# A state read turned one step later, and a state pass whose chunk splits move between the halves of a step

## The chip, the cores and the metric

The kernel runs on one core of a Trainium2 chip. The metric is the device time of one execution in microseconds (us); lower is better. The kernel before was run three times.

## The reference

Three stages follow each other; all of it is float32.

1. Attention between a sequence `x` (8 batches, 8 heads, 512 tokens, 64 wide) and a state of 32 rows per head: each token reads the states (`xread`), each state row reads the tokens (`sread`). Both are softmax attentions without projections. Together they give 8 x (512 + 32) = 4608 rows of 512.
2. A dense layer pair: `g = max(0.01 * h, h)` with `h = x @ w_in` (512 to 2048), then `g @ w_out` (2048 to 512).
3. A mixture of 8 experts (512 to 1024 to 512, relu) in which each row goes to the one expert of its largest logit; the result is scaled by the softmax weight and by a sigmoid gate.

```
h = x @ w_in ; g = maximum(0.01 * h, h) ; x = g @ w_out
logits = x @ w_gate ; e = argmax(logits) ; eom = sigmoid(x @ w_output_gate)
out = softmax(logits)[e] * eom[e] * (relu(x @ w1[e]) @ w2[e])
```

## The kernel before

**Numbers.** A float32 product is made from three matmuls of rounded parts: each operand is split into a `hi` part (a cast, made by ScalarE) and a `lo` part (operand minus `hi`, made by VectorE). `product` (L506 to L510) issues hi x lo, lo x hi and hi x hi. So each operand costs TensorE nothing, but ScalarE and VectorE one operation each, and TensorE waits for the `lo` part.

**Order of the work.** Each engine has one program written out by hand, and semaphores between them. There are nine layers, `layer(b)`: 0 to 7 are the batches with 512 tokens each, and layer 8 (`b == B`) is the state pass: the 256 state rows that the batches' attention left in `sread`. A layer has 16 steps f = 0 to 15, one for each 128 columns of the 2048. On TensorE a step is `up(b, f)` (or `up_states(f)` in the state pass), then `beside_up(b, f)`, then `down(b, f - 2)`, then `beside_down(b, f)`; after step 15 come down(14) and down(15). The two `beside` functions hold the small work of the neighbouring layers: the attention of the batch a = b + 1 and the routing of the rows of layer r = b - 1. The batches' W_in product is taken with the states first (`make_v`), so that `up` of a layer reads `v_hi`, `v_lo`, `aT_hi`, `aT_lo`; `up_states` has no such short cut and reads W_in itself, in 16 chunks of 128 columns, that are split on the way (`chunk_hi(f)` on ScalarE into `wch_hi`, L959, `chunk_lo(f)` on VectorE into `wch_lo`, L1337). `chunk_hi(f)` may start when up(f - 1) is done, and `up_states(f)` waits for `chunk_lo(f)`.

**The g step.** Behind up(f), ScalarE scales the bank by 0.01 (L937), VectorE takes the max (L1196, `g_ready`), ScalarE casts it into `gT_hi` (L943), and VectorE subtracts into `gT_lo` (L1200, `g_lo_done`), for which down(f) waits. up(f) waits for the max of f - 2. Both engines have a function `g_step`, with a `beside_g` between its halves; `layer` calls it and then does what belongs beside step f. In the state pass that is the routing of layer 7 (`keep_yT`, `keep_parts`, `exp_gates` on ScalarE; `add_logits`, `route`, `sum_gates`, `route_gate`, `route_ranks`, `route_rows`, `route_slots` on VectorE in steps 5 to 10), then the chunk f + 2, and then, in the steps of `FIRST_PIECE_AT` (0, 3, 11, 13), one piece of the first expert's weights (`split_expert`, L977 and L1333).

**The state read.** In step 13 of layer b TensorE makes the state read of batch a = b + 1 (`read_states`, L559) in `aux[0]`. VectorE copies it to `scT` (`keep_read`, L1163), TensorE turns it with two transposes into the other half of `aux[0]` (`turn_read`, L566), and VectorE copies that into `sread` (`keep_sread`, L1168 and L1169, `sread_kept`). For batch 0 this is done in steps 5 and 6 of layer 0. In step 15 TensorE waits for `sread_kept` and makes the next v in the same banks.

**The first expert's rows.** The routing sends the rows into a table in DRAM, ordered by expert. The expert with the most rows so far is chosen in layer 7 (`choose_first`), and GpSimd loads the first 256 of its rows into `xq` (`load_rows`, L413, `rows_in`) when the rows of layers 0 to 6 are in the table. In step 14 of the state pass VectorE waits for them and turns them with two transposes (`turn_quarters`, L1352) into `t_b`, the banks 2 and 3; the state pass uses banks 0 and 1 for its downs. It also copies their scales into `s_next`, which lies in a part of `y_buf` that the scatter of layer 7's rows still reads; that is what the wait for `rows_set` is for. After step 15 ScalarE and VectorE make `xgT_hi` and `xgT_lo` from `t_b` (L968, L1346), and the expert phase begins.

Of the kernel before, what the change touches and what calls it, by code (L numbers as in the profile page):

```python
# [35 lines left out]
def build(nc, xT_in, x_in, stT_in, st_in, w_in, w_out, w_gates, w1, w2, consts, tri_in, slot_init, out):  # L36
# [7 lines left out]
    with ctx:  # L44
# [460 lines left out]
        def _(pe):  # L505
# [163 lines left out]
            def beside_up(b, f):  # L669
# [10 lines left out]
                elif f == 3 and r is None:  # L680
                    flip_a2(0, 0, aux[0])
                elif f == 4 and r is None:
                    flip_a2(0, 1, aux[1])
                elif f == 6 and r is None:
                    turn_read(0)
                elif f == 4 and r is not None:
                    if b < B:
                        pe.wait_ge(v_lo_done, v_count(b, 1, 1))
                    else:
                        pe.wait_ge(yT_ready, 4 * r + 2)  # L690
                    flip_y(r, 3)
                elif f == 14 and a is not None:
                    turn_read(a)

            def beside_down(b, f):
# [44 lines left out]
                elif f == 13 and a is not None:  # L740
                    read_states(a)
                elif f == 15 and a is not None:
                    pe.wait_ge(sread_kept, a + 1)
                    make_v(a, 0)
# [135 lines left out]
        def _(act):  # L880
# [50 lines left out]
            def g_step(b, f):  # L931
# [5 lines left out]
                act.mul(g_buf[:, n, 0:w], up_b[n][:, 0:w], 0.01).then_inc(scaled, 1)  # L937
                beside_g(b, f)
                act.wait_ge(g_ready, u)

# [38 lines left out]
            def layer(b):  # L979
                a, r = b + 1 if b < B - 1 else None, b - 1 if b > 0 else None  # L980
                for f in range(F1):
# [24 lines left out]
                    if b == B - 1 and f == F1 - 1:  # L1006
                        chunk_hi(0)
                    if b == B and f + 2 < F1:
                        chunk_hi(f + 2)
                    if b == B and f in FIRST_PIECE_AT:  # L1010
# [82 lines left out]
        def _(dve):  # L1093
# [98 lines left out]
            def g_step(b, f):  # L1192
# [4 lines left out]
                if b < B - 1:  # L1197
                    beside_g(b + 1, f)
                dve.wait_ge(g_hi_done, u)
                dve.tensor_tensor(gT_lo[f % 4][:, 0:w], g_buf[:, n, 0:w], gT_hi[f % 4][:, 0:w].bitcast(fp32), ALU.subtract).then_inc(g_lo_done, 1)  # L1200
# [147 lines left out]

            def turn_quarters(i):
                dve.wait_ge(rows_in, 80 * i + 80)  # L1350
                for n in range(2):
                    dve.transpose(t_b[n][:, :].rearrange("p (k g t) -> p g k t", k=2, t=NS),  # L1352
                                  xq[:, :, 2 * NS * n:2 * NS * n + 2 * NS].rearrange("p g (k d) -> p g k d", k=2)).then_inc(t_ready, 1)
                if not (isinstance(i, int) and i == 0):
                    dve.wait_ge(s_moved, i)
                dve.wait_ge(t_ready, 2 * i + 2)
                dve.tensor_copy(s_next[:, :].rearrange("p (u o) -> p u o", o=1), s_in[:, :, 0:1]).then_inc(s_taken, 2 if isinstance(i, int) and i == 0 else 1)

            def layer(b):
                a, r = b + 1 if b < B - 1 else None, b - 1 if b > 0 else None  # L1360
                for f in range(F1):
# [43 lines left out]
                    if a is not None:  # L1405
# [3 lines left out]
                        elif f == 13:  # L1409
                            a_lo(a, 1)  # L1410
                            keep_read(a)
                        elif f == 14:
                            keep_sread(a)
                        elif f == 15:
                            v_rest(a, 0)
                    if r is not None and f == (14 if b < B else 10):
                        route_slots(r, 4)
                    if b == B and f == 14:
                        dve.wait_ge(y_kept_a, 2 * B)
                        dve.wait_ge(rows_set, 64 * B)  # L1420
                        turn_quarters(0)
                    if b == B - 1 and f == 0:
# [3 lines left out]
                    if b == B - 1 and f == F1 - 1:  # L1426
                        chunk_lo(0)
                    if b == B and f + 2 < F1:
                        chunk_lo(f + 2)
                    if b == B and f in FIRST_PIECE_AT:  # L1430
# [227 lines left out]
```

## Time and profile before

| | |
|---|---|
| median of 3 runs | 1134.91 us (1133.59 to 1134.99) |
| the profiled execution | 1132.32 us, span 1130.6 us |
| TensorE (PE) busy | 1107.4 us, 98% of the span |
| VectorE (DVE) busy | 624.0 us, 55% |
| ScalarE (ACT) busy | 401.5 us, 36% |
| GpSimd (POOL) busy | 206.9 us, 18% |
| granted TensorE clock, mean | 0.999 of full speed |
| state pass | about 648 to 700 us of the span |

In the rows below, times are us from the start of the span. PE is TensorE's matmuls, DVE VectorE, ACT ScalarE, POOL GpSimd. L508 is line 508 of the kernel. A timeline row has start, duration, engine, line, operation, what it writes and reads, sizes and the number of instructions merged; in brackets stands how long the engine was idle before it, and what released it. Matmuls overlap: one of 512 columns is shown as 0.39 us long, but the next starts 0.23 us after it, so distances are taken from start to start.

### The profile page before, as it was taken

How to read it: one execution, taken by the hardware profiler on the slowest of the kernel's cores; microseconds unless marked ns; L12 is line 12 of the kernel's file. 1: busy time of each engine (PE TensorE's matmuls, PEld its weight loads, DVE VectorE, ACT ScalarE, POOL GpSimd, SP SyncE). 2: the span in 40 equal slices, each digit the busy share in tenths (PEclk: the TensorE clock that was granted, in tenths of full speed). 3: DMA queues.
4: the chain of work that ended last, by engine and by line, in shares of the span. 5: the costliest groups of instructions: out<-in, count | busy, mean ns of one | idle time of the engine just before them, and what ended most of it. 6: DMA issues, size and time to landing. Idle time of an engine off the chain costs nothing.

```text
span 1130.6 us, 18025 instructions
## 1 busy us (share of the span) xinstructions
PE 1107.4 (98%) x6514; PEld 895.5 (79%) x6515; DVE 624.0 (55%) x1365; ACT 401.5 (36%) x752; POOL 206.9 (18%) x297
## 2 busy tenths in 40 slices
PE   6999999999999999999999999999999999999997
PEld 2777777777777777777777888998998988889895
DVE  6684574664754854844844566745333335467242
ACT  4344334334434433443343355333111124154121
POOL 1100011020020020110110303532222232443231
PEclk9999999999999999999999999999999999999999
DMA  9398297495693891940030301277111112645110
GB/s 339 130 287 242 76 279 213 126 281 159 181 291 95 233 284 52 289 127 1 38 75 1 131 2 38 86 196 189 46 46 56 37 60 70 178 102 146 41 54 23
DMA packets 73010, 149.87 MB, mean 133 GB/s; under 512 B 11232, under 2 KB 12512, under 8 KB 72929
## 3 DMA queue, kind: packets, MB, share of 16 engines
q1 hardware_dynamic: 59696, 115.34, 36.5%
q0 software_dynamic: 13248, 33.71, 10.3%
q8 instruction: 36, 0.59, 0.2%
q14 instruction: 30, 0.24, 0.1%
HBM read 131.11 MB, written 92.01 MB: 197 GB/s over the span
## 4 chain that ended last, share of the span: by engine, by line
PE 90%; DVE 5%; DMA 2%; issue 1%; ACT 1%; POOL 0%; DVEq 0%; SPq 0%; ACTq 0%; POOLq 0%
PE bank L508 28%; PE bank L510 27%; PE bank L509 26%; PE bank L541 3%; PE bank L559 2%; DMA raw<-w_dram 1%; PE bank L575 1%; DVE w_lo L1333 1%; PE bank L583 1%; PE bank L519 1%; PE bank L548 1%; DMA XT<-xT_in_dram 0%; DVE g_buf L1196 0%; PE bank L793 0%; DVE gT_lo L1200 0%
## 5 line engine op out<-in xcount | busy, mean ns | idle before, releaser
L508 PE MATMUL bank<-wout_lo,gT_hi 128*128 128x512 f32 x544 | 215.9, 397 | 1.4 <-DVE gT_lo L1200 0.9
L510 PE MATMUL bank<-wout_hi,gT_hi 128*128 128x512 f32 x544 | 212.3, 390 | 0.0
L509 PE MATMUL bank<-wout_hi,gT_lo 128*128 128x512 f32 x544 | 212.0, 390 | 0.0
L1196 DVE TENSOR_TENSOR g_buf<-g_buf,bank 128x512 f32<-128x512 f32 (+1 forms) x144 | 94.2, 655 | 102.9 <-ACT g_buf L937 100.8
L508 PE MATMUL bank<-xgT_lo,w_hi 128*128 128x256 f32 x512 | 144.7, 283 | 0.6 <-DVE w_lo L1333 0.5
L510 PE MATMUL bank<-xgT_hi,w_hi 128*128 128x256 f32 x512 | 143.8, 281 | 0.0
L509 PE MATMUL bank<-xgT_hi,w_lo 128*128 128x256 f32 x512 | 143.8, 281 | 0.0
L937 ACT ACTIVATE g_buf<-bank 128x512 f32<-128x512 f32 (+1 forms) x144 | 82.5, 573 | 150.0 <-PE bank L510 148.3
L1200 DVE TENSOR_TENSOR gT_lo<-g_buf,gT_hi 128x512 fp32r<-128x512 f32 (+1 forms) x144 | 95.4, 662 | 72.9 <-ACT gT_hi L943 70.9
L404 POOL DMA_INDIRECT rows_dram<-y_buf,row_i x34 | 35.0, 1030 | 543.2 <-DVE row_i L1290 535.5
L943 ACT CAST gT_hi<-g_buf 128x512 fp32r<-128x512 f32 (+1 forms) x144 | 85.9, 597 | 134.3 <-DVE g_buf L1196 132.6
L1034 ACT ACTIVATE hT_hi<-bank 128x256 fp32r<-128x256 f32 x128 | 49.1, 383 | 220.6 <-PE bank L510 218.3
L508 PEld LDWEIGHTS bank<-wout_lo,gT_hi 128*128 128x128 f32 x544 | 102.2, 188 | 28.1 <-DVE gT_lo L1200 6.4
L510 PEld LDWEIGHTS bank<-wout_hi,gT_hi 128*128 128x128 f32 x544 | 102.1, 188 | 22.4
L509 PEld LDWEIGHTS bank<-wout_hi,gT_lo 128*128 128x128 f32 x544 | 102.3, 188 | 20.2
L508 PE MATMUL bank<-w_lo,hT_hi 128*128 128x512 f32 x296 | 116.4, 393 | 0.7
L510 PE MATMUL bank<-w_hi,hT_hi 128*128 128x512 f32 x296 | 115.5, 390 | 0.0
L509 PE MATMUL bank<-w_hi,hT_lo 128*128 128x512 f32 x296 | 115.5, 390 | 0.0
L508 PE MATMUL bank<-aT_lo,v_hi 128*128 128x512 f32 x254 | 107.9, 425 | 0.8 <-DVE v_lo L1178 0.2
L1463 DVE SCALAR_TENSOR_TENSOR hT_lo<-bank,hT_hi 128x256 fp32r<-128x256 f32 x128 | 53.4, 424 | 87.4 <-ACT hT_hi L1034 83.7
L510 PE MATMUL bank<-aT_hi,v_hi 128*128 128x512 f32 x254 | 100.1, 394 | 0.0
L509 PE MATMUL bank<-aT_hi,v_lo 128*128 128x512 f32 x254 | 99.7, 392 | 0.0
(217 smaller groups left out, 1740.8 us busy)
## 6 DMA issues: line engine op xcount, KB each, us to landing
rows_dram<-x_in_dram SPq DMA_DIRECT2D x17, 4128.0 KB
xq<-rows_dram POOLq DMA_DIRECT2D x88, 128.0 KB, 2.9
raw<-w_dram SPq DMA_DIRECT2D x20, 512.0 KB
raw<-w_dram SPq DMA_DIRECT2D x10, 1024.0 KB
X<-x_in_dram SPq DMA_DIRECT2D x8, 1024.0 KB
XT<-xT_in_dram SPq DMA_DIRECT2D x7, 1024.0 KB, 5.7
win<-w_in_dram SPq DMA_DIRECT2D x4, 1024.0 KB, 13.0
y_buf<-w_out_dram POOLq DMA_DIRECT2D x6, 512.0 KB, 6.5
```

Source lines behind the costliest of these rows:

```text
L404: pool.indirect_dma_start(out=rows_dram, out_offset=bass.IndirectOffsetOnAxis(ap=row_i[:, t:t + 1], axis=0), in_=y_buf[:, t, :], in_offset ...
L508: pe.matmul(o, l_hi, r_lo, start=first, stop=False)
L509: pe.matmul(o, l_lo, r_hi, start=False, stop=False)
L510: return pe.matmul(o, l_hi, r_hi, start=False, stop=last)
L541: last = pe.matmul(to[g][NS * c:NS * c + NS, :], stT[b % 2][rows, c, cols], win[rows, c, VW * k:VW * k + VW], start=True, stop=True)
L559: last = pe.matmul(aux[0][D * i:D * i + D, P * u:P * u + P], a_flat[:, q:q + 2 * NS], X[:, t, P * c:P * c + P], start=(t == 0), stop=(t == 3))
L937: act.mul(g_buf[:, n, 0:w], up_b[n][:, 0:w], 0.01).then_inc(scaled, 1)
L943: act.copy(gT_hi[f % 4][:, 0:w], g_buf[:, n, 0:w]).then_inc(g_hi_done, 1)
L1034: act.activation(hT_hi[:, f, :], h_b[f % 4][:, :PAIR], ACT.Relu).then_inc(h_hi_done, 1)
L1196: dve.tensor_tensor(g_buf[:, n, 0:w], g_buf[:, n, 0:w], up_b[n][:, 0:w], ALU.max).then_inc(g_ready, 1)
L1200: dve.tensor_tensor(gT_lo[f % 4][:, 0:w], g_buf[:, n, 0:w], gT_hi[f % 4][:, 0:w].bitcast(fp32), ALU.subtract).then_inc(g_lo_done, 1)
L1463: dve.scalar_tensor_tensor(hT_lo[:, f, :], h_b[f % 4][:, :PAIR], 0.0, hT_hi[:, f, :].bitcast(fp32), ALU.max, ALU.subtract).then_inc(h_lo_d ...
```

## The change

Three edits.

1. `turn_read(a)` for the batches 1 to 7 moves from `beside_up(b, 14)`, ahead of down(12), to `beside_down(b, 14)`, behind it. On VectorE `route_slots` now comes ahead of `keep_sread` in step 14.
2. In the state pass (the first `g_step` of the diff is ScalarE's, the second VectorE's) `chunk_hi(f + 2)` moves from the end of step f into ScalarE's `g_step`, between the scaling and the cast, and `chunk_lo(f + 2)` into VectorE's, between the max and gT_lo.
3. `turn_quarters` is divided into `turn_tiles` and `take_scales`. In the state pass the transposes of the first expert's rows are done at the end of step 4, the scales are still taken in step 14. Elsewhere `turn_quarters` calls both.

```diff
             def beside_up(b, f):
...
-                elif f == 14 and a is not None:
-                    turn_read(a)
...
             def beside_down(b, f):
...
                     read_states(a)
+                elif f == 14 and a is not None:
+                    turn_read(a)
...
             def g_step(b, f):
...
                 beside_g(b, f)
+                if b == B and f + 2 < F1:
+                    chunk_hi(f + 2)
                 act.wait_ge(g_ready, u)
...
-                    if b == B and f + 2 < F1:
-                        chunk_hi(f + 2)
...
             def g_step(b, f):
...
                     beside_g(b + 1, f)
+                if b == B and f + 2 < F1:
+                    chunk_lo(f + 2)
                 dve.wait_ge(g_hi_done, u)
...
-            def turn_quarters(i):
+            def turn_tiles(i):
                 dve.wait_ge(rows_in, 80 * i + 80)
                 for n in range(2):
                     dve.transpose(...).then_inc(t_ready, 1)
+
+            def take_scales(i):
                 if not (isinstance(i, int) and i == 0):
                     dve.wait_ge(s_moved, i)
                 dve.wait_ge(t_ready, 2 * i + 2)
                 dve.tensor_copy(s_next[...], s_in[:, :, 0:1]).then_inc(s_taken, ...)
+
+            def turn_quarters(i):
+                turn_tiles(i)
+                take_scales(i)
...
-                        elif f == 14:
+                    if r is not None and f == (14 if b < B else 10):
+                        route_slots(r, 4)
+                    if a is not None:
+                        if f == 14:
                             keep_sread(a)
                         elif f == 15:
                             v_rest(a, 0)
-                    if r is not None and f == (14 if b < B else 10):
-                        route_slots(r, 4)
                     if b == B and f == 14:
-                        dve.wait_ge(y_kept_a, 2 * B)
                         dve.wait_ge(rows_set, 64 * B)
-                        turn_quarters(0)
+                        take_scales(0)
...
-                    if b == B and f + 2 < F1:
-                        chunk_lo(f + 2)
+                    if b == B and f == 4:
+                        dve.wait_ge(y_kept_a, 2 * B)
+                        turn_tiles(0)
```

## Rows read from the trace of the kernel before

**Rows 1.** TensorE's waits of the whole span: engine, line, releaser: us, times, longest.
```profile
PE bank L566 <- DVE scT L1163: 0.9, 5, 0.2
PE bank L508 <- DVE gT_lo L1200: 0.9, 1, 0.9
PE bank L508 <- DVE wch_lo L1337: 0.7, 2, 0.5
```
**Rows 2.** Timeline of TensorE around the turned state read, layer 6.
```profile
560.62 0.39 PE L510 MATMUL bank<-aT_hi,v_hi 128*128 128x512 f32 x1
561.16 0.44 PE L566 MATMUL bank<-const,scT 128*128 128x128 f32 x2 [0.15 <-issue]
...
561.67 0.39 PE L509 MATMUL bank<-wout_hi,gT_lo 128*128 128x512 f32 x1
```
**Rows 3.** Timeline of TensorE around the same transposes, layer 0.
```profile
85.16 0.39 PE L510 MATMUL bank<-aT_hi,v_hi 128*128 128x512 f32 x1
85.39 0.38 PE L566 MATMUL bank<-const,scT 128*128 128x128 f32 x2
...
85.84 0.40 PE L509 MATMUL bank<-wout_hi,gT_lo 128*128 128x512 f32 x1
```
**Rows 4.** Timeline of VectorE, layer 6, the copy before the transposes.
```profile
560.68 0.42 DVE L1163 COPY scT<-bank 128x256 f32<-128x256 f32 x1 [2.16 <-PE bank L559]
```
**Rows 5.** Timeline of TensorE in the state pass, around its stalls.
```profile
652.12 0.35 PE L508 MATMUL bank<-sr_lo,wch_hi 128*128 128x256 f32 x1 [0.50 <-DVE wch_lo L1337]
...
655.22 0.40 PE L510 MATMUL bank<-wout_hi,gT_hi 128*128 128x512 f32 x1
655.62 0.35 PE L508 MATMUL bank<-sr_lo,wch_hi 128*128 128x256 f32 x1
...
672.07 0.39 PE L510 MATMUL bank<-wout_hi,gT_hi 128*128 128x512 f32 x1
672.52 0.36 PE L508 MATMUL bank<-sr_lo,wch_hi 128*128 128x256 f32 x1
...
678.15 0.39 PE L510 MATMUL bank<-wout_hi,gT_hi 128*128 128x512 f32 x1
678.74 0.35 PE L508 MATMUL bank<-sr_lo,wch_hi 128*128 128x256 f32 x1 [0.20 <-DVE wch_lo L1337]
678.93 0.28 PE L509 MATMUL bank<-sr_hi,wch_lo 128*128 128x256 f32 x1
...
696.99 0.39 PE L510 MATMUL bank<-wout_hi,gT_hi 128*128 128x512 f32 x1
698.31 0.50 PE L508 MATMUL bank<-wout_lo,gT_hi 128*128 128x512 f32 x1 [0.93 <-DVE gT_lo L1200]
```
**Rows 6.** Timeline of ScalarE, step 0 of the state pass.
```profile
649.45 0.38 ACT L937 ACTIVATE g_buf<-bank 128x256 f32<-128x256 f32 x1 [0.81 <-PE bank L510]
650.32 0.41 ACT L943 CAST gT_hi<-g_buf 128x256 fp32r<-128x256 f32 x1 [0.49 <-DVE g_buf L1196]
650.63 0.62 ACT L959 CAST wch_hi<-win 128x512 fp32r<-128x512 f32 x1
```
**Rows 7.** Timeline of VectorE in the state pass: chunks, a split, the row transposes.
```profile
651.28 0.69 DVE L1337 TENSOR_TENSOR wch_lo<-win,wch_hi 128x512 fp32r<-128x512 f32 x1
...
683.53 0.69 DVE L1337 TENSOR_TENSOR wch_lo<-win,wch_hi 128x512 fp32r<-128x512 f32 x1
...
693.08 1.23 DVE L1333 TENSOR_TENSOR w_lo<-raw,w_hi 128x1024 fp32r<-128x1024 f32 x1 [0.26 <-issue]
...
695.45 1.31 DVE L1352 STREAM_TRANSPOSE bank<-xq 128x512 f32<-128x512 f32 x2
```
**Rows 8.** GpSimd: row loads, a row scatter, and the loads' landing (queries xq, timeline).
```profile
645.05 2.40 POOL L413 DMA_DIRECT2D xq<-rows_dram  x4
...
682.83 1.02 POOL L404 DMA_INDIRECT rows_dram<-y_buf,row_i  x1 [0.31 <-issue]
...
DMA to landing us min/median/max: 2.7/2.8/2.9
```

## The prediction

> **What bounds the kernel now.** I read the list of TensorE's waits first, because in a kernel whose matmul engine is busy all the time only what stops that engine can be won. In the eight layers it names one repeated wait, that of the two state-read transposes for the copy that feeds them, 0.9 us in five places; in the state pass it names one for gT_lo (0.9 us) and two for wch_lo (0.7 us) [rows 1]. The other waits of that list lie in the first 75 us or in the expert phase, where the diff changes nothing. So TensorE sets the end, and the question is how much of its time between these places is stall. A wait costs more than its idle number, because the matmuls behind it start anew; I therefore read the timeline of TensorE at each place and take distances from start to start. An undisturbed 512-column matmul is followed by the next instruction 0.23 us after its start (85.16 to 85.39) [rows 3].
>
> **Part one, the state read.** Now TensorE runs up(14), then the transposes, then down(12). The copy L1163 that they need starts at 560.68 and takes 0.42 us [rows 4], while the last matmul of up(14) has already started at 560.62; the transposes start at 561.16. From that last up matmul to the second down matmul there are 561.67 - 560.62 = 1.05 us [rows 2]. Layer 0 shows the same four instructions without a wait (there the copy was early): 85.84 - 85.16 = 0.68 us [rows 3]. The difference, 0.37 us, is the price of one wait with its restart. The transposes stand in seven layers (0 to 6); layer 0 already pays nothing, so six remain: 6 x 0.37 = 2.2 us. Their idle time is 0.15 us in layer 6, but 0.9 us over the five others, 0.18 each [rows 1, 2], so I add 5 x 0.03 and round to **2.4 us**.
>
> After the change the transposes come behind down(12), 12 matmuls of 0.23 us (2.7 us) later than now, when the copy has long ended: nothing waits, and the two transposes cost what layer 0 shows. What is moved by this: the copy into sread on VectorE waits for them. VectorE first does route_slots, which has been put ahead of it and has nothing to do with the transposes; its eight small operations now stand behind the copy. The copy must be over before TensorE's make_v of step 15, another up and down (12 + 6 matmuls, over 4 us) behind the transposes, and before VectorE's own max of step 15. I cost it at nothing; its cover is that up and down. If it were gone, the two copies (under 1 us) would stall TensorE once a layer.
>
> **Part two, the state pass.** One step is 12 matmuls of 256 columns and 6 of 512, about 2.8 us. Five stalls are in the diff's reach [rows 5]:
> up(2) idles 0.50 us for its chunk;
> 655.62 - 655.22 = 0.40, less 0.23, is 0.17;
> 672.52 - 672.07 = 0.45, so 0.22;
> 678.74 - 678.15 = 0.59, so 0.36;
> 698.31 - 696.99 = 1.32, so 1.09, before the last down.
> Together 2.34 us. After a wait the next start is late too: 678.93 - 678.74 = 0.19 where half of 0.23 would do, 0.07 us more. Five times that is 0.35. Sum 2.7 us; since the first stall follows transposes, its own restart may be dearer, and I take **2.8 us**, with 2.3 (idle alone) and 3.0 as bounds.
>
> Are they removed? The first four are chunks that come late. ScalarE starts the scaling of step 0 at 649.45, casts g at 650.32 and only then the chunk at 650.63; VectorE subtracts it from 651.28 and TensorE starts at 652.12 [rows 5, 6, 7]. Between the chunk's two halves there are 0.65 us, from the second to TensorE 0.84, and from one ScalarE operation of this size to the next 0.31. In the new order the chunk starts right behind the scaling: 649.45 + 0.31 + 0.65 + 0.84 = 651.25, and TensorE comes there at 652.12 - 0.50 = 651.62, or, if the restart is counted in, some 0.2 earlier. So it is just in time; this is the tightest place, and a remainder of 0.1 or 0.2 us is possible. The other chunks have more: since the chunk now goes ahead of what a step does beside it (the route, the gates, the splits of the first expert, 1.23 us each [rows 7]), it is ready some 1.8 us after the scaling starts, while TensorE needs it only after two downs and an up, over 4 us. Those side jobs no longer hold up a chunk, only the next max.
>
> The last stall has another cause. Around 693 to 698 VectorE is one queue: a split of 1.23 us from 693.08, max and gT_lo of step 14, then the two transposes of the first expert's rows, 1.31 us from 695.45, and only then max and gT_lo of step 15, for which TensorE waits 1.09 us [rows 5, 7]. The change takes the 1.31 us out of this queue and moves it to step 4; only the small copy of the scales stays. 1.31 is more than 1.09, and the split before it also comes earlier, because the chunk ahead of it does; so the whole stall goes.
>
> What it adds: a step's cast and gT_lo now stand behind the chunk on their engines. On VectorE the chunk's 0.69 us comes between max and gT_lo, of which some 0.5 us was spent waiting for the cast; gT_lo is 0.2 us later, 0.7 us where ScalarE also copies a transposed y. The down that reads it is two steps away, more than 3 us of room; in steps 14 and 15 there is no chunk at all. I cost it at nothing. The row transposes at step 4 stand behind gT_lo(4) and ahead of max(5): 1.31 us in a step of 2.8 us that also holds one split; max(5) may be late, but what needs it is up(7). They wait for the rows, whose loads are issued from 645.05 in 2.4 us and land 2.8 us later [rows 8], so by about 651; step 4 is reached after 660. The bound from below is nothing, from above the time by which the loads would be later than 660. Banks and buffers that they write lie unused in this pass. The order of GpSimd's queue is the same; its row scatters start 1 to 2 us earlier with the gates.
>
> **The sum.** 2.4 + 2.8 = 5.2 us. After the state pass each chain that TensorE takes part in starts from it (the last routing, the second rows, the loads of the experts, issued as buffers come free), so the shift should reach the end whole. The profiled execution took 1132.32 us (span 1130.6); it would be 1127.1. It is 2.6 us below the median of the runs shown; from the median 1134.91 the same 5.2 us (0.46%) give 1129.7.
>
> **The rivals.**
> *Chunks or turns stay late, one part alone pays.* If the state pass only moves its stalls (each engine does as much as before, and 0.2 us at up(2) is thin), only 2.4 us remain: 1132.5. If instead the transposes behind down(12) make something else in the layer late, 2.8 us remain: 1132.1. For the first speaks that VectorE is fuller here than in a layer; against it that each of the five stalls has its own named operation in front, which is moved.
> *No change that can be told.* The layers and the pass both just move the wait to the next place, for example to gT_lo before a down. The room of over 3 us speaks against it. 1134.9.
> *Slower: the rows aren't there.* At step 4 VectorE waits for the row loads; all that stands behind it (max(5), the chunks) then holds up TensorE. It decides once the loads land later than about 664, 13 us later than the rows say [rows 8]; from there each us costs one, and beyond 5.2 more it is slower than before: with the landing at 675, some 11 - 5 = 6 us, 1141. In the kernel before this would have been hidden, since it waited for them at 695.
> *GpSimd and VectorE block each other.* The row scatters of GpSimd move against VectorE's two-input subtractions. The row says no: a scatter from 682.83 lasts 1.02 us, and the chunk's subtraction at 683.53, inside it, takes 0.69 us as does the one at 651.28 with GpSimd idle [rows 7, 8]. If a new meeting did cost a whole scatter, 1.0 us in a step that also has a split, I would lose about 1 us: 1130.7.
> The Trainium skill, "SBUF — State Buffer", section "Who interferes with whom", has the rule for this rival: a VectorE instruction with two SBUF inputs contends with a GpSimd instruction that reads SBUF, and the loser waits the whole instruction. By that rule the sum would be 4.2 instead of 5.2; the trace does not show it at the one meeting that I read.
>
> **How the numbers follow.** Forecast 0.72; one part alone 0.13; GpSimd's blocking 0.03; no change 0.08; slower 0.04. A change of 0.2% (2.3 us) is about what a measurement of this kernel can tell from none. The forecast and the blocking case are beyond it; one part alone, 2.4 or 2.8 us, comes out beyond it in some seven of ten: faster 0.72 + 0.03 + 0.09 = 0.84, within 0.12, slower 0.04. The range goes from all bounds at their best (2.4 + 3.0, and another 1.3 us, by which the lowest run shown lies under the median) at 1128.2 to one part alone at 1132.6.
>
> **What the profile after would show.** TensorE's waits without the state-read transposes, and 0.68 us in layers 1 to 6 where 1.05 stood, one down later; no wait for gT_lo and at most a short one for wch_lo at up(2); the row transposes on VectorE near 661; the expert phase as before, 5 us earlier. I am wrong if TensorE waits for gT_lo before a down in the state pass, if make_v waits for sread in every layer, or if VectorE idles at step 4 for a load.

## The result, and the profile after

The changed kernel takes 1127.24 us (median of 4 runs, 1126.89 to 1127.44), the kernel before in the same comparison 1134.66 us (4 runs, 1133.59 to 1134.99). The ratio is 0.9938, with a 95% interval of 0.9925 to 0.995: it is 7.4 us faster, 0.6%; in us the interval is 5.7 to 8.5. The forecast was 1129.7 us with a range from 1128.2 to 1132.6, so the time lies below the range. The two profiled executions are 5.4 us apart: 1132.32 to 1126.89 us, spans 1130.6 to 1125.2 us. The one of the changed kernel is one of its four timed runs; that of the kernel before is not among its four and lies 1.3 us below the lowest of them, and whether it ran on the same chip is not known.

First the list of TensorE's waits after the change (releaser, us in total, times, longest), to be laid beside [rows 1]:

```profile
core 0 of [0], span 1125.2 us
PE bank L532 <- DMA stT<-stT_in_dram: 5.3, 1, 5.3
PE bank L616 <- ACT aT_hi L899: 2.4, 2, 2.0
...
PE bank L508 <- DVE w_lo L1335: 0.5, 1, 0.5
PE bank L508 <- DVE hT_lo L1472: 0.3, 1, 0.3
PE bank L541 <- DVE sread L1169: 0.3, 1, 0.3
```

All three rows of [rows 1] are gone: no wait of the transposes for scT, none for wch_lo, none for gT_lo. The wait for sread was there before with the same 0.3 us. One is new, 0.3 us for hT_lo in the expert phase, at 1031.69. It is no mark of the change: later profiles of the kernel before have it too, `control` with 0.4 us and `control_2` with 0.6.

**The state read.** The trace's answer on the sixteen transposes after the change: duration in ns (least, median, most), first and last start, then what ended idle time before them, and who waited for them. Both lists are empty.

```profile
L566 PE MATMUL bank<-const,scT x16: 270/271/273, 44.6 to 561.5; 128*128 128x128 f32 x16
its engine sat idle before it (us, times) until:
who waited for it (us, times):
```

In each of the layers 0 to 6 the last matmul ahead of the transposes and the second down matmul behind them are 0.68 us apart, the distance of [rows 3]. In [rows 2] it was 1.05. But the copy that feeds them is no earlier. VectorE after, layer 6:

```profile
555.63 0.68 DVE L1173 TENSOR_TENSOR aT_lo<-scT,aT_hi 128x512 fp32r<-128x512 f32 x1
559.18 0.42 DVE L1163 COPY scT<-bank 128x256 f32<-128x256 f32 x1 [2.87 <-remote]
559.89 0.69 DVE L1196 TENSOR_TENSOR g_buf<-g_buf,bank 128x512 f32<-128x512 f32 x1 [0.28 <-ACT g_buf L937]
```

The state read begins at 555.25 on TensorE, the copy 3.9 us later, after VectorE had idled for 2.9 us. The late copy now has down(12) in front of its reader.

**The state pass.** (It has 256 rows; with the 8 x 512 of the batches the kernel works on 4352, and the 4608 in the section on the reference is a slip: 8 x (512 + 32) is 4352.) TensorE around up(2), where [rows 5] show a start at 652.12 with 0.50 us of waiting:

```profile
648.34 0.28 PE L510 MATMUL bank<-sr_hi,wch_hi 128*128 128x256 f32 x1
648.46 0.60 PE L575 MATMUL bank<-const,y_buf 128*128 128x128 f32 x4
648.81 0.36 PE L508 MATMUL bank<-sr_lo,wch_hi 128*128 128x256 f32 x1
```

The timeline of ScalarE in that step, which answers to [rows 6]:

```profile
646.89 0.39 ACT L937 ACTIVATE g_buf<-bank 128x256 f32<-128x256 f32 x1 [0.81 <-PE bank L510]
647.17 0.61 ACT L961 CAST wch_hi<-win 128x512 fp32r<-128x512 f32 x1
647.77 0.41 ACT L945 CAST gT_hi<-g_buf 128x256 fp32r<-128x256 f32 x1
```

And that of VectorE, for [rows 7], with step 4 behind it:

```profile
647.31 0.42 DVE L1196 TENSOR_TENSOR g_buf<-g_buf,bank 128x256 f32<-128x256 f32 x1 [0.50 <-ACT g_buf L937]
647.82 0.69 DVE L1339 TENSOR_TENSOR wch_lo<-win,wch_hi 128x512 fp32r<-128x512 f32 x1
...
658.66 0.68 DVE L1339 TENSOR_TENSOR wch_lo<-win,wch_hi 128x512 fp32r<-128x512 f32 x1
659.26 0.42 DVE L1202 TENSOR_TENSOR gT_lo<-g_buf,gT_hi 128x256 fp32r<-128x256 f32 x1
659.60 1.31 DVE L1354 STREAM_TRANSPOSE bank<-xq 128x512 f32<-128x512 f32 x2
661.93 0.42 DVE L1196 TENSOR_TENSOR g_buf<-g_buf,bank 128x256 f32<-128x256 f32 x1 [1.03 <-ACT g_buf L937]
```

The chunk starts 0.28 us behind the scaling (before: 1.18, 649.45 to 650.63) and its second half 0.93 us behind it (before: 1.83). The row transposes run at step 4 without a wait for their rows, and VectorE idles 1.03 us behind them, so they had room. The end of the pass, where [rows 5] show 1.32 us between two starts:

```profile
693.75 0.39 PE L509 MATMUL bank<-wout_hi,gT_lo 128*128 128x512 f32 x1
693.97 0.39 PE L510 MATMUL bank<-wout_hi,gT_hi 128*128 128x512 f32 x1
694.20 0.28 PE L508 MATMUL bank<-xgT_lo,w_hi 128*128 128x256 f32 x1
```

Nothing but steps of 0.23 us, up to the first matmul of the expert phase. So the gain can be read off at fixed places of TensorE's program. The first wait of the kernel's L541 ends 0.26 us earlier (48.32 to 48.06), before any edited place. up(1) of the state pass begins at 646.96 instead of 649.51: 2.55 us, so the seven layers gave 2.29. The expert phase begins at 694.20 instead of 699.82: 5.62, so the state pass gave 3.07. The spans end 5.4 us apart; the expert phase gave 0.2 back, where the profile after has the wait for hT_lo.

By this the working holds against the profiled execution: 2.4 was forecast for the turns and 2.29 came, 2.8 for the pass and 3.07 came, just above its bound of 3.0; 1127.1 was the time and 1126.89 it was. What does not hold is the median: 7.4 us, where the parts give 5.4. The experiments ask where the other 2 us are, and why the copy of the state read is late at all.

### The profile page after: what moved, and what is told of

Its sections match the earlier page's. It is cut to its first block, busy times and chain, and to the rows that moved or that the text cites. A ratio compares the mean times of both kernels' runs of the same rounds, so it can differ in the third digit from the quotient of the medians.

```text
span 1125.2 us, 18025 instructions
## 1 busy us (share of the span) xinstructions
PE 1103.7 (98%) x6514; PEld 895.9 (80%) x6515; DVE 622.4 (55%) x1365; ACT 401.2 (36%) x752; POOL 207.6 (18%) x297
## 4 chain that ended last, share of the span: by engine, by line
PE 91%; DVE 4%; DMA 2%; issue 1%; ACT 1%; POOL 0%; DVEq 0%; SPq 0%; ACTq 0%; POOLq 0%
PE bank L508 29%; PE bank L510 27%; PE bank L509 27%; PE bank L541 3%; PE bank L559 1%; DMA raw<-w_dram 1%; PE bank L575 1%; PE bank L583 1%; PE bank L519 1%; PE bank L548 1%; DVE w_lo L1335 1%; DMA XT<-xT_in_dram 1%; DVE v_lo L1178 0%; PE bank L793 0%; PE bank L590 0%
## 5 line engine op out<-in xcount | busy, mean ns | idle before, releaser
L937 ACT ACTIVATE g_buf<-bank 128x512 f32<-128x512 f32 (+1 forms) x144 | 82.5, 573 | 153.8 <-PE bank L510 152.2
```

## The experiments

Each kernel was timed beside the kernel before on the same chip. The kernels of one table were timed together on one chip, and that is called one comparison here; with the one above there are seven. A median's ratio has an interval of about 0.1% to either side, 1 us.

### The three edits apart (second comparison; before: 1131.46 us, 33 runs)

`control` is the kernel before, unchanged. `turn_only` has edit 1 of the diff, `chunks_only` edit 2, `rows_only` edit 3. Their core:

```diff
 turn_only
-                elif f == 14 and a is not None:      # beside_up
-                    turn_read(a)
+                elif f == 14 and a is not None:      # beside_down
+                    turn_read(a)
 chunks_only
+                if b == B and f + 2 < F1:            # in both g_step
+                    chunk_hi(f + 2)                  # chunk_lo on VectorE
 rows_only
-                        turn_quarters(0)             # step 14
+                        take_scales(0)
+                    if b == B and f == 4:
+                        dve.wait_ge(y_kept_a, 2 * B)
+                        turn_tiles(0)
```

> The kernel before, under another name. Theory A (the gain is 5.4 us, the difference of the two profiled spans, and the other 2 us of the medians is a spread of executions that has nothing to do with the change): the control's own runs spread over 1132 to 1135, ratio 0.9985 to 1.0015, and with five rounds the median of before may come down to 1133. Theory B (the executions of the kernel before without the luck of the profiled one are really 2 us longer, because its stalls are longer there): runs at 1134 to 1135 with few exceptions.

> Only the state read's transposes behind down(12), with route_slots ahead of keep_sread. By the profile 6 x 0.39 = 2.3 us less, TensorE without the wait for L1163; in the medians 2.3 us as well by theory A. By theory B, if the stalls in the layers are what differs between executions, up to 4 us.

> Only the chunk splits between the halves of the g step. The stalls at up(2), up(3), up(8), up(10) go (1.7 us); the wait for gT_lo before the last down stays but is shorter, since the split ahead of the row transposes comes some 0.5 us earlier: 2.0 to 2.4 us less in all. The rival that the stalls move to a down would leave it at 0 to 1 us.

> Only the transposes of the first expert's rows in step 4. The wait before the last down goes, 1.2 us less; the four chunk stalls stay, and the one or two chunks behind step 4 may come later, since they now stand behind 1.31 us of transposes: a gain between 0.7 and 1.2 us. If it interacts with the chunks (max of step 5 late, chunk 7 late) 0 to 0.5 us.

| kernel | median us | ratio, 95% interval | against 1131.46 |
|---|---|---|---|
| control | 1131.68 | 1.0004, 0.9995 to 1.0013 | +0.2 |
| turn_only | 1129.84 | 0.9985, 0.9976 to 0.9994 | -1.6 |
| chunks_only | 1129.36 | 0.9984, 0.9975 to 0.9993 | -2.1 |
| rows_only | 1131.24 | 0.9999, 0.999 to 1.0008 | -0.2 |

`chunks_only` came as expected, the others did not. The kernel before is itself 3.2 us faster here than in the first comparison (1131.46 against 1134.66). `turn_only` gained 1.6 us where 2.3 or more were expected. And the rows' edit, which by [rows 5] should have been worth 1.09 us, is worth nothing that can be told. The end of the state pass of `control` says why:

```profile
696.13 0.39 PE L510 MATMUL bank<-wout_hi,gT_hi 128*128 128x512 f32 x1
696.51 0.50 PE L508 MATMUL bank<-wout_lo,gT_hi 128*128 128x512 f32 x1
```

0.38 us between the starts, so a stall of 0.15 and not of 1.09, in the same program. The stalls of the chunks are as in [rows 5]: 0.75 us at up(2) with its restart, 0.16, 0.21 and 0.36. The turns of the state read are cheaper too: 1.03, 0.94, 0.91, 0.91, 0.95 and 0.95 us in the layers 1 to 6 of `control`, where 0.68 is the undisturbed distance. The excess is 1.6 us, and `turn_only` gains 1.6 in the median (0.7 to 2.7 by its interval); in `turn_only` all seven are 0.68.

### The whole, and the whole less one part (third comparison; before: 1129.74 us, 33 runs)

`full_again` is the changed kernel. `turn_chunks` leaves the rows where they were, `state_only` leaves out edit 1, `turn_no_slots` leaves route_slots behind keep_sread.

```diff
 turn_no_slots, against the changed kernel, VectorE, step 14
-                    if r is not None and f == (14 if b < B else 10):
-                        route_slots(r, 4)
                     if a is not None:
...
+                    if r is not None and f == (14 if b < B else 10):
+                        route_slots(r, 4)
```

> The whole change, timed together with the kernel before. Theory C (the price of the removed waits is that which this chip's executions show, 0.25 us a turn and 0.2 us before the last down where these are as in the control's profile): the parts alone gave 1.6, 2.1 and 0.2 us, so 3.7 to 4.0 us in all. Theory A (5.4 us, as between the first two profiles): 5.2 to 5.6. Theory B (7.4 us, as between the first medians): above 7.

> The change without the early row transposes. Theory C: the two parts add, 3.7 us, and the rows add nothing to it, because the earlier chunks already free the end of VectorE's queue. The rival (the row transposes' 1.31 us at the end of the pass are worth 1 us): 1 us slower than the whole change, with a wait for gT_lo before the last down.

> Chunks and rows without the turned state read. Theory C: as the chunks alone, 2.1 to 2.3 us. The rival that the two help each other (rows at step 4 were held up by late chunks): 3 us or more.

> The whole change, but route_slots stays behind keep_sread on VectorE. By my forecast nothing, within 0.3 us of the whole change, since over 4 us of matmuls lie between the transposes and the make_v that needs the copy. The rival: VectorE waits 0.5 us or so for the later transposes, is late with the max of step 15, and that costs 0.3 us or more in each of six layers, 2 us or more.

| kernel | median us | ratio, 95% interval |
|---|---|---|
| full_again | 1127.68 | 0.9983, 0.9974 to 0.9992 |
| turn_chunks | 1127.89 | 0.9984, 0.9975 to 0.9993 |
| state_only | 1127.59 | 0.9981, 0.9972 to 0.999 |
| turn_no_slots | 1127.75 | 0.9982, 0.9973 to 0.9991 |

The four can't be told apart and are some 2.1 us faster than before; the 3.7 us or more that were expected of `full_again` and `turn_chunks` did not come. On this chip the turned read is worth nothing: `state_only`, which hasn't got it, shows 0.68 us in every layer. The order of route_slots is worth nothing, as costed, and the early row transposes 0.2 us, which can't be told from nothing. And the changed kernel takes 1127.7 us, close to the 1127.2 of the first comparison, while the kernel before has gone from 1134.7 over 1131.5 to 1129.7. What varies from comparison to comparison is the kernel before.

### The cause of the late copy (fourth comparison; before: 1129.46 us, 27 runs)

`control_2` and `full_3` repeat both kernels. `scatter_late` holds back GpSimd's row scatters of the layers 0 to 5 until the state read is kept; `copy_act` lets ScalarE make the copy L1163.

```diff
 scatter_late, GpSimd
-            with pool.Fori(1, B) as blocks:
+            for blocks in range(1, B - 1):
+                pool.wait_ge(sread_kept, blocks + 2)
 copy_act, ScalarE, beside step 13 (VectorE's keep_read(a) is left out)
+                        elif f == 13:
+                            act.wait_ge(sread_ps, a + 1)
+                            act.wait_ge(aT_lo_done, 2 * a + 1)
+                            act.copy(scT[:, 0, 0:2 * P], aux[0][:, 0:2 * P]).then_inc(read_kept, 1)
```

> The kernel before once more, for a profile of it from the chip of this call. In its profiles so far the copy L1163 of layers 1 to 6 starts 3.1 to 3.3 us after the state read's first matmul, while in layer 0, and in every layer of the four kernels of the last call, it starts 2.0 us after. Theory D (the row scatters that GpSimd issues at that moment hold the copy back on some chips and not on others): either 2.0 and no turn stall with a time of before near 1129.7, or 3.1 or more with a stall of 0.25 us or more a turn and a time of 1131 or more. Nothing in between.

> The whole change. Theory D: its own time is 1127.0 to 1127.9 on any chip, since it waits for none of the things that differ; the gain is the kernel before's time less that: 2.0 us where before takes 1129.7, 4 where it takes 1131.5, 7.4 where it takes 1134.7. The rival (chips differ for reasons outside the stalls, and both kernels alike): the gain stays near 2 to 4 whatever the kernel before takes.

> The kernel before, in which GpSimd issues the row scatters of the batches' layers 0 to 5 only after the state read of the layer is kept. Theory D: the copy starts 2.0 us after the first state-read matmul in layers 1 to 6 and the turns cost 0.68 us as in layer 0, on any chip; where the kernel before has the stall, 1.5 to 2.4 us less, otherwise the same time. The rival (the lateness has nothing to do with the scatters): 3.1 us and the stall stay.

> The kernel before, in which ScalarE instead of VectorE copies the read states of layers 0 to 6. If it is VectorE that the scatters hold back, the copy on ScalarE starts 2.0 to 2.1 us after the first matmul in every layer, and the turn stall goes (1.5 to 2.4 us less where it is). If the signal from TensorE is late for everybody, the copy is late on ScalarE too, with the stall unchanged.

| kernel | median us | ratio, 95% interval |
|---|---|---|
| control_2 | 1129.59 | 1.0, 0.999 to 1.0009 |
| full_3 | 1127.36 | 0.9979, 0.997 to 0.9988 |
| scatter_late | 1147.23 | 1.0157, 1.0138 to 1.0175 |
| copy_act | 1130.33 | 1.0007, 0.9998 to 1.0016 |

`full_3` lies in the 1127.0 to 1127.9 us that were expected of it on any chip. This chip, too, has no late copy to cure, and so neither of the two could decide. But it gives the undisturbed picture of the place of [rows 2, 4]. The timeline of TensorE in `control_2`, the kernel before, layer 6:

```profile
555.48 1.75 PE L559 MATMUL bank<-X,a_buf 128*64 128x128 f32 x28
...
558.64 0.39 PE L510 MATMUL bank<-aT_hi,v_hi 128*128 128x512 f32 x1
558.87 0.38 PE L566 MATMUL bank<-const,scT 128*128 128x128 f32 x2
559.01 0.48 PE L508 MATMUL bank<-wout_lo,gT_hi 128*128 128x512 f32 x1
559.32 0.40 PE L509 MATMUL bank<-wout_hi,gT_lo 128*128 128x512 f32 x1
```

And that of VectorE there:

```profile
555.87 0.68 DVE L1173 TENSOR_TENSOR aT_lo<-scT,aT_hi 128x512 fp32r<-128x512 f32 x1
557.50 0.42 DVE L1163 COPY scT<-bank 128x256 f32<-128x256 f32 x1 [0.94 <-PE bank L559]
```

The copy starts 2.02 us behind the first matmul of the read, in this and every other layer; in the first profile it was 560.68 - 557.46 = 3.22 us. In neither is VectorE busy when the read ends: the copy only waits for TensorE's signal. The records of the semaphores say the same from the other side. They hold the time at which each increment was made; from the start of the last matmul of the state read to the increment that releases the copy, the median over the eight reads is

```
kernel before, first profile      1.52 us
kernel before, control            1.38 us
kernel before, control_2          0.30 us
changed kernel, full_again        0.30 us
```

So it is the signal itself that is late, by some 1.2 us, and not VectorE that is busy. (The ends of matmuls are modelled in a profile, so it can't say whether the last matmul's result came late as well; the matmuls behind it started on time.) In the first profile the same holds at v_ps (some 1.2 us late in each of the layers 1 to 6), at the up of one later step of each layer (0.4 us) and at three ups of the state pass, its steps 12 to 14 (1.1, 1.3 and 1.5 us). Of these the timeline of ScalarE shows the last two in the first profile and in `control_2`, at the scaling (L937) that the signal releases. First the kernel before, first profile:

```profile
690.29 0.38 ACT L937 ACTIVATE g_buf<-bank 128x256 f32<-128x256 f32 x1 [1.22 <-PE bank L510]
...
693.31 0.38 ACT L937 ACTIVATE g_buf<-bank 128x256 f32<-128x256 f32 x1 [0.26 <-remote]
```

Then `control_2`, ScalarE as well:

```profile
686.60 0.38 ACT L937 ACTIVATE g_buf<-bank 128x256 f32<-128x256 f32 x1
...
689.56 0.38 ACT L937 ACTIVATE g_buf<-bank 128x256 f32<-128x256 f32 x1
```

The last matmul of up(14) starts at 691.41 in the one and at 689.09 in the other, so the scaling follows 1.90 us behind it in the one and 0.47 in the other. That shifts VectorE's queue at the end of the pass. Its row transposes start at 695.45 [rows 7] in the one, at 692.06 in the other: 3.39 us apart, while TensorE is only 2.4 us apart there. The 1.0 us between is the difference of the last stall: 1.09 us in the first profile, 694.92 - 694.55 - 0.23 = 0.14 in `control_2`. In `control` up(12) and up(14) are late as well, by 1.0 and 0.6 us, but not up(13); its row transposes start where those of `control_2` do, seen from TensorE (693.65, and the matmul ahead of the stall at 696.13), and its last stall is 0.15 us. So of these two profiles the late signals of the pass cost something only in the one in which up(13) is among them.

`copy_act` is 0.9 us above the kernel before, which its interval does not tell from none. `scatter_late` was 17.8 us slower (5 runs) for another reason than the one under test: the next layer's y waits for the late scatters, and TensorE for y.

```profile
184.87 0.63 PE L578 MATMUL bank<-const,y_buf 128*128 128x128 f32 x4 [3.68 <-DVE y_buf L1210]
```

### Are GpSimd's scatters the cause? (three more comparisons)

The late signals fall in the parts of a layer in which GpSimd issues the scatters of rows and slots. GpSimd's timeline in the first profile, layer 6, the last row scatter beside the state read of [rows 4]:

```profile
559.67 0.98 POOL L404 DMA_INDIRECT rows_dram<-y_buf,row_i  x1 [0.30 <-issue]
```

It ends at 560.65; the read's increment, due 0.30 us behind its last matmul at 559.45, is recorded at 560.66, and the copy starts at 560.68. In the other five layers too the increment comes within 0.03 us of the end of a row scatter. Over the whole profile, past its first 30 us, 26 of TensorE's increments are over 0.15 us later than is usual for their semaphore, and each of them is made while GpSimd is at an indirect scatter or within 0.4 us of it (80 of the 615 increments are); the profile after has 21 and `control` 24, all in such places. `no_scatter` leaves those of six layers out, for small ordinary DMAs that raise the same semaphores (the slots' in the same way as the rows' below); part of the table stays empty. `control_3` to `control_5` stand beside it.

```diff
-            with pool.Fori(1, B) as blocks:
-                set_rows(blocks, 4)
-                set_slots(blocks, 4)
+            for b in range(1, B - 1):
+                pool.wait_ge(row_ready, b)
+                for t in range(4):
+                    pool.dma_start(pad_dram[8 * b + t:8 * b + t + 1, :], row_i[0:1, 0:4]).then_inc(rows_set, 16)
+...
```

> The kernel before once more, unchanged, for its profile on this chip: ratio 1.000. It says whether TensorE's completion signals are late here. If they are, the last up matmul stands 0.9 to 1.1 us from the second down matmul in the layers 1 to 6 at step 14, and the copy behind the state read starts some 3.2 us after that read's first matmul; if they are not, 0.68 us and 2.0 us, and the time should lie near 1129.5.

> The kernel before, but GpSimd's indirect scatters of the rows and of their slots are left out for the layers 0 to 5; in their place it writes 16 bytes with an ordinary DMA each, which raises the same semaphores. This part of the table stays empty, so the output isn't the reference's; the work of the other engines is the same. Theory A (the scatters make TensorE's signals late): on a chip where the kernel before has late signals, the layers 1 to 6 show 0.68 us from the last up matmul to the second down matmul and 2.0 us from the state read to its copy, and the kernel is 1.6 to 4 us faster than before. Theory B (the lateness belongs to the chip and meets the same places whatever GpSimd does): 0.9 to 1.1 us and 3.2 us stay, and the time is within 0.5 us of before. Where the kernel before has no late signals, both give 0.68 and the same time, and the run tells nothing.

> The kernel before, unchanged, for its profile on this chip: ratio 1.000. Late completion signals of TensorE show as 0.9 to 1.1 us from the last up matmul to the second down matmul in the layers 1 to 6, and 3.2 us from the state read to its copy; none, as 0.68 and 2.0 us.

> As no_scatter, again on another chip. If the kernel before has late signals here: 0.68 and 2.0 us and 1.6 to 4 us faster by theory A (the scatters cause them), 0.9 to 1.1 and 3.2 us and no difference over 0.5 us by theory B (the chip's own). If it has none, the run tells nothing.

> The kernel before, unchanged, for its profile on this chip: ratio 1.000. Late completion signals of TensorE show as 0.9 to 1.1 us from the last up matmul to the second down matmul in the layers 1 to 6, and 3.2 us from the state read to its copy; none, as 0.68 and 2.0 us.

> As no_scatter, a last time on another chip. If the kernel before has late signals here: 0.68 and 2.0 us and 1.6 to 4 us faster by theory A, 0.9 to 1.1 and 3.2 us and no difference over 0.5 us by theory B. If it has none, the run tells nothing.

| comparison | before us | control | no_scatter |
|---|---|---|---|
| 5 (chip 1) | 1129.63 | 1129.48 | 1129.92, ratio 1.0004 (0.9994 to 1.0013) |
| 6 (chip 0) | 1129.47 | 1129.57 | 1129.45, ratio 0.9999 (0.9989 to 1.0009) |
| 7 (chip 1 again) | 1129.82 | 1129.63 | 1129.89, ratio 1.0 (0.999 to 1.001) |

All three controls show 2.0 us from the read to the copy, and, past the first 30 us, no signal that is late by more than 0.15 us: the lateness that costs time was not there, and for it the question stays open. But there is a small one. The increment of step 15's v (L541), 0.67 us behind the start of its last matmul everywhere else, comes 0.06 to 0.09 us later than that in 17 of the 24 layers 1 to 6 of `control_2` to `control_5` (12 of 18 on the chips of the `no_scatter` runs), where it is due 0.5 us after a slot scatter has begun. In the three `no_scatter` profiles it is never late (18 layers), and not in `full_again`, `full_3` and `turn_chunks` either, where it is due behind the end of a scatter. So the scatters do make such a signal late, by under 0.1 us and at no cost here; that the lateness of 1.2 us has the same cause is likely by its places, not shown. The runs also tell how common the large one is: two of the seven comparisons had it. In the five others, on four chips, the kernel before takes 1129.5 to 1129.8 us.

## Why the prediction missed

**What bounds the kernel; the five stalls and the turns; their removal.** Right. Each place named is free of its wait in the profile after, and no new wait came in the layers or the pass. The forecast 5.2 us is 5.4 between the profiled executions.

**Part one, the state read.** The 0.37 us a layer was read rightly and came back, 2.29 of 2.4. It is not the program's own, though: 1.6 us in a second comparison (shown by `turn_only` and its control) and nothing in the other five (`state_only` and the controls, all at 0.68). The row that could have said so is [rows 4]: VectorE had been idle for 2.16 us with nothing else to do before that copy, and the profile put the wait down to the state read. The prediction took the copy's start as given and did not ask why it came more than 3 us after the read began.

**Part two, the chunks.** Right in mechanism, size and place: four stalls, 1.25 us of idle by the prediction's own figures [rows 5], 1.5 with the dearer restart at up(2); `chunks_only`, which also loses the last stall of 0.15 us, measured 2.1, with an interval of about 1 us to either side. up(2), the tightest place, has no remainder. The chunk's second half was forecast 0.96 us behind the scaling and came 0.93 behind it.

**The last stall.** Here the cause was half wrong. "The last stall has another cause. Around 693 to 698 VectorE is one queue": the queue is there in every comparison, but it costs 0.15 us. The other 0.95 are the late signals of the steps 12 to 14, which push the queue back. The change removes the whole of it. Which edit does so is not shown: `chunks_only` has no last stall either, but was only profiled where it was 0.15 us, and no run with two of the edits met the stall of 1.09.

**The step that failed** is in the sum: "It is 2.6 us below the median of the runs shown; from the median 1134.91 the same 5.2 us (0.46%) give 1129.7." That takes the distance from the profiled execution to the median for a thing that the change does not touch. But most of that distance went with the change. After the change that distance is 0.35 us (1126.89 to 1127.24) where it was 2.34 (1132.32 to 1134.66), and 5.4 + 2.34 - 0.35 = 7.4. So the term that was mis-sized is the whole gain from the median, 5.2 us where 7.4 were measured (5.7 to 8.5). The range took the same step again: it allowed 1.3 us for the spread of the runs, where the profiled execution already lay 1.3 us below the lowest of the four. That these 2 us are more late signals in the timed executions is argued, not shown: each kernel has a profile of only one execution in a comparison, and the first profile of the kernel before is of an execution outside the four. Another cause of the 2 us, a profile taken on another chip among them, is not ruled out. For the late signals speaks that the changed kernel takes 1127.2 to 1127.7 us in all three comparisons in which it ran, with the late signals (in its own first profile the read's copy is still 3.2 to 3.9 us behind) and without, and that the kernel before differs there by 5 us; and that the parts in the second comparison, 1.6 + 2.1 + 0.2 = 3.9 us (each within about 1 us), lead from its 1131.5 to the same 1127.6. The size of the gain was luck of the comparison in either case: in the quiet ones, without the large lateness, the same forecast of 5.2 us would have met 2.1.

**The rivals.** One part alone, no change and the missing rows did not come about in the first comparison. In the two quiet ones that have the changed kernel "one part alone pays" is what is measured: 2.1 us, for the reason that the turns have nothing to win there, and not because something else became late. The blocking of GpSimd and VectorE is not seen on VectorE's side, but it is there on GpSimd's. All sixteen subtractions of the chunks take 681 to 694 ns before and 681 to 693 ns after the change, inside a scatter or not.

```profile
L1339 DVE TENSOR_TENSOR wch_lo<-win,wch_hi x16: 681/692/693, 640.7 to 685.6; 128x512 fp32r<-128x512 f32 x16
```

The scatters do not keep their length. Timelines of VectorE and of GpSimd, two rows of before, then two of after the change:

```profile
686.50 1.22 DVE L1333 TENSOR_TENSOR w_lo<-raw,w_hi 128x1024 fp32r<-128x1024 f32 x1 [0.26 <-issue]
686.72 1.86 POOL L396 DMA_INDIRECT slots_dram<-r_int  x1 [0.30 <-issue]
...
681.39 1.22 DVE L1335 TENSOR_TENSOR w_lo<-raw,w_hi 128x1024 fp32r<-128x1024 f32 x1 [0.43 <-ACT w_hi L979]
681.78 1.69 POOL L404 DMA_INDIRECT rows_dram<-y_buf,row_i  x1 [0.31 <-issue]
```

Each of these two scatters begins while VectorE is at a subtraction with two inputs in SBUF, with 1.00 and 0.83 us of it to go, and is 0.88 and 0.71 us longer than the usual 0.98. The row and slot scatters of the first profile, the profile after and `control_2` all follow that. 47 begin with over 0.15 us of such a subtraction to go, and 46 of these are longer by what is left of it less 0.12 us, to 0.02; the other 157 take 0.97 to 1.07 us. This agrees with the rule of the Trainium skill, "SBUF — State Buffer", section "Who interferes with whom", with GpSimd as the loser; the rule's other half, a VectorE subtraction that begins inside a scatter and loses, does not show. The one meeting that the prediction read could not show it: that scatter had begun 0.70 us before the subtraction, which outlasts it by 0.37 [rows 7, 8]. "No" was right for VectorE, and the rival's price, 1.0 us lost, did not come about, because what waited was GpSimd and TensorE waits for none of its scatters there.

## What to carry to other kernels

Where the profiled execution lies outside the timed ones, the difference is part of the question: ask which stalls could make it up, and whether the change removes them too, before a gain is carried from one to the other. When an engine idles for a producer that by its distance from the last instruction should have signalled already, compare the time of the increment with that in another profile of the same program: the length of such a wait need not be a property of the program. A step of other work between that signal and its reader covers it. Here an edit that gains nothing in a quiet comparison, the turned read, gained 1.6 us in one that was not, and the kernel with all three edits took 1127.2 to 1127.7 us in each of the three in which it ran.

## What the runs showed of the hardware

- The same program differs by 0.5% between comparisons: 1129.5 to 1129.8 us in five of them (four chips), 1131.5 and 1134.7 in the two others. The granted clock is 0.996 to 0.999 in all profiles and does not order them. That the difference belongs to the chip is not shown: the one chip that was met twice was quiet both times, no chip with late signals was met again, and the chip of the first comparison is not known.
- TensorE's completion signals came some 1.2 us late at a read's end (1.9 us in layer 6 of the profile after) and let a scaling start 1.9 us behind its last matmul, at mostly the same places of the program in the two comparisons that had this. All of them coincide with GpSimd's indirect scatters, one in the expert phase included. In the quiet comparisons one signal a layer was 0.06 to 0.09 us late inside a scatter in most layers of the controls (once 0.22 us, in `turn_no_slots`), and in none of three profiles without the scatters. That the scatters cause the large lateness is open; it would need `no_scatter` beside its control where the large lateness is, and of the six comparisons behind the first only the second had it, in which `no_scatter` did not run.
- An indirect scatter that GpSimd begins during a VectorE subtraction with two SBUF inputs takes longer by what is left of the subtraction less 0.12 us (46 of 47 in three profiles), up to 0.88 us; the subtraction keeps its length.
- The length of a wait, then, can vary while the idle time that a late operation of the program causes does not: 0.50 us for wch_lo at up(2) and 0.20 at up(10) stand in each profile of the kernel before, in all six comparisons that have one.
